# Seven products in place of eight in the second feed-forward layer's up projection

## The reference

```python
def _moe2_ref(x, w_in, w_out, g_ln):       # x: 3072 x 512, w_in: 512 x 1024, w_out: 1024 x 512
    h = x @ w_in
    h_max = np.max(h, axis=-1, keepdims=True)
    e = np.exp(h - h_max)
    sm = e / (np.sum(e, axis=-1, keepdims=True) + 1e-09)
    solu = h * sm
    mu = np.mean(solu, axis=-1, keepdims=True)
    var = np.mean((solu - mu) ** 2, axis=-1, keepdims=True)
    ln = (solu - mu) / np.sqrt(var + 1e-06) * g_ln
    return (ln @ w_out).astype(np.float32)

def reference(...):
    attn_out = _attn_ref(...)               # q, k, v: 4 x 8 x 768 x 64
    x = ...                                 # tokens by features: 3072 x 512
    x = _moe_ref(x=x, ...)                  # gate and value: 512 x 1536 each, out: 1536 x 512
    return _moe2_ref(x=x, ...)
```

## Time and profile before

| | us |
|---|---|
| median of three runs | 971.77 |
| the profiled execution's own time | 974.78 |
| its span, first to last instruction | 972.9 |
| PE busy in the span | 941.5 (97%) |
| DVE busy | 643.6 (66%) |
| ACT busy | 521.7 (54%) |
| POOL busy | 136.1 (14%) |
| stage C, from 697 to the end | 276 |

### The profile page before, as it was taken

One profiled execution on the slowest core, in us unless ns is written; L12 is line 12 of the kernel. 1 busy time (PEld: TensorE's weight loads), 2 busy tenths in 40 slices (PEclk: granted clock), 3 DMA queues, 4 the chain that ended last, 5 costly groups with the idle time before them and its releaser, 6 DMA issues.

```text
span 972.9 us, 14652 instructions
## 1 busy us (share of the span) xinstructions
PE 941.5 (97%) x5334; PEld 832.9 (86%) x5334; DVE 643.6 (66%) x1065; ACT 521.7 (54%) x911; POOL 136.1 (14%) x170
## 2 busy tenths in 40 slices
PE   7979999999999999999999999999999999999996
PEld 4666787787799999999999999999988888888875
DVE  3767885786778755454568877777475775666641
ACT  3554654555555533342546554555477876666632
POOL 4313401101115330000044001010100000000000
PEclk9989999999999999999999999999999999999999
DMA  9746635626153413131374617250520154351533
GB/s 264 215 155 201 183 153 174 184 115 182 55 210 120 157 71 130 49 115 66 111 247 143 229 52 248 87 191 17 170 75 32 27 137 96 88 141 34 112 86 84
DMA packets 103847, 126.61 MB, mean 130 GB/s; under 512 B 8160, under 2 KB 84320, under 8 KB 103776
## 3 DMA queue, kind: packets, MB, share of 16 engines
q1 hardware_dynamic: 98320, 109.28, 36.6%
q0 software_dynamic: 4736, 15.73, 4.7%
q10 hardware_dynamic: 720, 0.66, 0.3%
HBM read 77.41 MB, written 37.75 MB: 118 GB/s over the span
## 4 chain that ended last, share of the span: by engine, by line
PE 79%; DVE 7%; DMA 4%; issue 3%; ACT 3%; SPq 2%; POOL 2%; DVEq 0%; ACTq 0%; POOLq 0%
PE psum L949 10%; PE psum L952 10%; PE psum L951 10%; PE psum L385 8%; PE psum L386 8%; PE psum L387 8%; PE psum L985 6%; PE psum L987 6%; PE psum L988 6%; PE psum L842 3%; PE psum L876 2%; PE psum L866 2%; PE psum L855 2%; DMA w_raw<-weights 1%; DMA v_buf<-v_rows 1%
## 5 line engine op out<-in xcount | busy, mean ns | idle before, releaser
L949 PE MATMUL psum<-xo_hi,w_hi 128*128 128x384 f32 x560 | 195.1, 348 | 7.8 <-DVE psum L1658 2.6
L951 PE MATMUL psum<-xo_lo,w_hi 128*128 128x384 f32 x560 | 188.3, 336 | 0.0
L952 PE MATMUL psum<-xo_hi,w_lo 128*128 128x384 f32 x560 | 188.1, 336 | 0.0
L949 PEld LDWEIGHTS psum<-xo_hi,w_hi 128*128 128x128 f32 x560 | 105.8, 189 | 13.9 <-DVE xo_lo L1644 4.1
L951 PEld LDWEIGHTS psum<-xo_lo,w_hi 128*128 128x128 f32 x560 | 105.9, 189 | 0.8 <-issue 0.3
L952 PEld LDWEIGHTS psum<-xo_hi,w_lo 128*128 128x128 f32 x560 | 105.8, 189 | 0.0
L1163 ACT ACTIVATE xo_hi<-b 128x768 fp32r<-128x768 f32 x84 | 70.6, 846 | 63.2 <-PE psum L988 49.5
L1538 DVE TENSOR_TENSOR xo_lo<-b,xo_hi 128x768 fp32r<-128x768 f32 x84 | 81.2, 969 | 34.5 <-ACT xo_hi L1163 34.3
L385 PE MATMUL psum<-w_out_hi,ln_t_hi 128*128 128x512 f32 x192 | 75.1, 391 | 2.1 <-DVE ln_t_lo L1775 2.1
L1658 DVE TENSOR_TENSOR psum<-psum,p_buf 128x384 f32<-128x384 f32 x48 | 27.1, 564 | 75.0 <-PE psum L952 75.0
L385 PE MATMUL psum<-w_in_hi,x_hi 128*128 128x512 f32 x192 | 75.3, 392 | 0.4 <-ACT h_buf L1284 0.4
(11 more groups left out here) (142 smaller groups left out, 2025.2 us busy)
## 6 DMA issues: line engine op xcount, KB each, us to landing
act_dram<-act_buf SPq DMA_DIRECT2D x48, 384.0 KB, 2.4
b<-act_dram SPq DMA_DIRECT2D x48, 384.0 KB, 4.9
ln_t<-z SPq DMA_DIRECT2D x80, 128.0 KB, 3.1
kq_buf<-k_t SPq DMA_DIRECT2D x32, 192.0 KB, 2.7
kq_buf<-q_t SPq DMA_DIRECT2D x64, 96.0 KB, 3.0
q_dec<-q_t SPq DMA_DIRECT2D x32, 192.0 KB, 2.5
w_raw<-weights POOLq DMA_DIRECT2D x12, 512.0 KB, 4.4
x_dram<-x_tile SPq DMA_DIRECT2D x4, 1536.0 KB, 6.0
```

What stands on the lines that cost most here:

```text
L949: pe.matmul(dst, hi[:, cols], xo_hi[:, i, kc, :], start=i in (P1, P7) and kc == 0, stop=False, skip_group_check=True)
L951: pe.matmul(dst, hi[:, cols], xo_lo[:, i, kc, :], start=False, stop=False, skip_group_check=True)
L952: mm = pe.matmul(dst, lo[:, cols], xo_hi[:, i, kc, :], start=False, stop=kc == HK - 1, skip_group_check=True)
```

## The change

The last seven pairs of blocks (k = 0 to 6, the first is blocks (2,2) and (2,3)) get their up projection by seven products of half size: tokens in two halves (the two blocks), features in two halves, columns in two halves of 512. A product is 2 slices x 3 = 6 matmuls of 512 columns, a pair 42 in place of 48. For it:

- POOL makes four sums of input blocks for each pair (`make_s`, four operations of 128x256, each waiting for the one before), and once, during the gated layer's second round of down products, four sums of weight blocks in eight pieces of 128x512, each stored to DRAM (`sum_t`); the pieces are loaded again by POOL's queue in stage C (`load_t`), two stages of 128x512, and split by ACT and DVE into four weight operands (`t_high`, `t_low`): pieces 0 to 3 in tile 0, pieces 4 to 7 inside the first pair.
- The split of a pair's inputs covers 1792 columns in place of 1024, in three parts (512, 256, 1024).
- PE takes the order P1, P7, P6, P2, P5, then the down projection of one block, then P3, P4, then the down projection of the next. ACT copies P1 from one PSUM bank to another between P1 and P6 (`copy_xy`), and P7 to SBUF (`copy_p7`); DVE adds for P5 and P4 (`add_u3`) and makes one quarter of the result (`add_c22`); ACT copies the other three (`copy_up`).
- Both blocks of a pair are then taken on together: two maxima, two exponents, two normalizations and transposes in a row. One turn buffer `z` holds a tile in place of two.

The core of the diff:

```diff
+        UP_ORDER = (P1, P7, P6, P2, P5, P3, P4)
+        T_PIECES = [(p, a) for p in (P7, P6, P5, P4) for a in range(HK)]
...
+            def up_product(k, i):
+                if i in (P1, P2):
+                    pe.wait_ge(s_lo_ready, 3 * k + 1)
+                else:
+                    pe.wait_ge(s_lo_ready, 3 * k + 3)
+                if k == 0 and i in (P4, P5, P6, P7):
+                    pe.wait_ge(t_lo_ready, T_PIECES.index((i, HK - 1)) + 1)
...
+                elif i in (P6, P2):
+                    pe.wait_ge(up_xy_copied, k + 1)
+                elif i in (P5, P4):
+                    pe.wait_ge(up_u3_ready, k + 1)
+                else:
+                    pe.wait_ge(up_c22_ready, k + 1)
...
                 for j in range(BLOCKS):
-                    if run_up_of(t, j):
-                        both_up(*run_up_of(t, j))
+                    if pair_up(t, j) is not None:
+                        for i in UP_ORDER[0:5] if j % 2 == 0 else UP_ORDER[5:7]:
+                            up_product(pair_up(t, j), i)
                     both_down2(t, j)
...
+            def load_t(i):                       # POOL
+                if i > 1:
+                    pool.wait_ge(t_lo_ready, i - 1)
+                pool.dma_start(t_stage(i)[:], t_store(i)).then_inc(t_loaded[i % 2], DMA)
...
+                    if j % 2 == 0:               # ACT, tiles 1 to 4
+                        if j > 0:
+                            scale_out(t, j - 1)
+                        elif t > 1:
+                            scale_out(t - 1, 3)
+                        ln_high(t, j, 0)
+                        copy_xy(k)
+                        ln_high(t, j, 1)
+                        if k == 0:
+                            for i in (4, 5):
+                                t_high(i)
+                        copy_p7(k)
+                        if k == 0:
+                            for i in (6, 7):
+                                t_high(i)
+                        square_solu(*last_of(k))
+                        deviation_of_pair(last_of(k)[0], last_of(k)[1] // 2)
+                        copy_up(k, P2, UX, 0, 0, up_c11_copied)
+                        if k + 1 < PAIRS:
+                            s_high(k + 1, 0)
+                        continue
                     both_high(t, j)
+                    scale_out(t, j - 1)
+                    copy_up(k, P3, UY, 0, 1, up_c12_copied)
+                    copy_up(k, P4, UV, 1, 0, up_c21_copied)
+                    exponent(*a)
+                    if k + 1 < PAIRS:
+                        s_high(k + 1, 1)
+                        s_high(k + 1, 2)
+                    else:
+                        both_high(*next_block(t, j))
+                    exponent(*b)
+                    square_solu(*a)
...
                     both_low(t, j)
+                    if j % 2 == 0:               # DVE, tiles 1 to 4
+                        if k == 0:
+                            for i in (4, 5):
+                                t_low(i)
+                        add_u3(k)
+                        invert_pair(last_of(k)[0], last_of(k)[1] // 2)
+                        add_c22(k)
+                        turn_up(last_of(k)[0], last_of(k)[1] - 1)
+                        turn_up(*last_of(k))
+                        if k == 0:
+                            for i in (6, 7):
+                                t_low(i)
+                        if k + 1 < PAIRS:
+                            s_low(k + 1, 0)
+                        continue
```

More of the change, by code:

```diff
@@ L227, in retention_moe_kernel @@
             squares = sb(c, "squares", [P, F2])
-            x2_hi0 = sb(c, "x2_hi0", [P, KC, 2 * P], F32R)
+            with ExitStack() as pair:
+                x2_hi0 = sb(pair, "x2_hi0", [P, KC, 2 * P], F32R)
+            up_p7 = sb(c, "up_p7", [P, BANK])
+            sb(c, "gap5", [P, 2 * KC * P - BANK])
             h_buf = sb(c, "h_buf", [P, 2, F2])
@@ L336, in retention_moe_kernel @@
         ln_t_moved = [sem(f"ln_t_moved{i}") for i in range(PARTS)]
+        t_summed = sem("t_summed")
+        t_stored = sem("t_stored")
+        b22_loaded = sem("b22_loaded")
+        t_loaded = [sem(f"t_loaded{i}") for i in range(2)]
+        t_hi_ready = sem("t_hi_ready")
+        t_lo_ready = sem("t_lo_ready")
+        s_made = sem("s_made")
+        s_hi_ready = sem("s_hi_ready")
+        s_lo_ready = sem("s_lo_ready")
+        up_product_done = sem("up_product_done")
+        up_xy_copied = sem("up_xy_copied")
+        up_p7_copied = sem("up_p7_copied")
+        up_u3_ready = sem("up_u3_ready")
+        up_c22_ready = sem("up_c22_ready")
+        up_c11_copied = sem("up_c11_copied")
+        up_c12_copied = sem("up_c12_copied")
+        up_c21_copied = sem("up_c21_copied")
         std_ready = sem("std_ready")
@@ L1019, in up @@
                 mm.then_inc(h_done, 1)
+            def up_product(k, i):
[5 more added lines that the diff above has]
+                    pe.wait_ge(t_lo_ready, T_PIECES.index((i, HK - 1)) + 1)
+                if i == P1:
+                    at_least(pe, up_c11_copied, k)
+                elif i == P7:
+                    at_least(pe, up_c21_copied, k)
+                elif i in (P6, P2):
+                    pe.wait_ge(up_xy_copied, k + 1)
+                elif i in (P5, P4):
+                    pe.wait_ge(up_u3_ready, k + 1)
+                else:
+                    pe.wait_ge(up_c22_ready, k + 1)
+                dst = psum[:, {P1: UX, P2: UX, P7: UV, P4: UV}.get(i, UY), :]
+                for a in range(HK):
+                    x_hi, x_lo = s_hi[:, S_OF[i] * HK + a, :], s_lo[:, S_OF[i] * HK + a, :]
+                    m_hi, m_lo = up_weight(i, a)
+                    pe.matmul(dst, x_hi, m_hi, start=i in (P1, P7) and a == 0, stop=False, skip_group_check=True)
+                    pe.matmul(dst, x_hi, m_lo, start=False, stop=False, skip_group_check=True)
+                    mm = pe.matmul(dst, x_lo, m_hi, start=False, stop=a == HK - 1, skip_group_check=True)
+                mm.then_inc(up_product_done, 1)
             def turn(t, j):
@@ L1314, in square_solu @@
                 act.wait_ge(mean_ready, n + 1)
+                act.wait_ge(squares_summed, {4: 2, 5: 3, 6: 3, 7: 3}.get(n, 4))
                 at_least(act, d_squared, n - BLOCKS)
                 at_least(act, pair_std_ready, 2 * (t - 2) + j // 2 + 1)
-                act.activation(d_squares[:], solu[:, j % 2, :], ACT.Square, bias=mean[:, one],
+                act.activation(squares[:], solu[:, j % 2, :], ACT.Square, bias=mean[:, one],
                                accum_out=squares_sum[:, one]).then_inc(d_squared, 1)
@@ L1423, in stage_c @@
                     copy_h(2, 0, 0)
-                    x2_high(2, 1)
+                    for part in range(3):
+                        s_high(0, part)
                     copy_h(2, 0, 1)
@@ L1864, in stage_c @@
                     take_up(1, 3)
-                    x2_low(2, 1)
+                    for part in range(3):
+                        s_low(0, part)
                     row_max(2, 0)
```

248 lines of the change are left out of this document (203 added, 45 removed).

## The result

With the change the kernel takes 981.46 us, the median of four runs (979.80, 980.24, 982.68, 982.79), against 972.14 for the kernel before in the same comparison: a ratio of 1.0091, with a 95% interval of 1.0067 to 1.0114. It moved by 9.3 us where I had forecast 4.3; the sign was right, and 981.46 lies above the upper end of my range, 980.8.

The account below looks back on a forecast made before the run. PE was taken to bound stage C, though waits set the end. Saved matmuls -9.5, steady pairs +2.5, first pair +8.2, tail +3.1 gave +4.3 us: 971.77 to 976.1 us, range 972.8 to 980.8.

Parts of the forecast that it names:

- The gain: Stage C on PE: seven pairs lose 6 matmuls each, 42 x 0.227 = 9.5 us saved if no new wait appears.
- the 9 that I named as a sign: Profile after the change: PE busy time lower by some 9 us, while stage C is longer by 4.
- The steady pairs: Six steps between pairs: P6 waits for ACT's copy of P1, 0.42 us a pair with restart, 2.5 us in all.
- P6, P5 and P4 of the first pair: PE waits in the first pair for ACT's copy, DVE's sum and the last weight piece: late by 2.4, 1.1 and 3.9 us.
- P3: First pair: P3's sum waits behind ACT's root, which stands behind pieces 6 and 7; late by 0.9 us.
- my own upper bound: First pair's net cost at most 11 us, if turned-block DMAs slow loads by 2 us and POOL's sums slow DVE.
- a cover for POOL's sums: POOL's eight weight sums are hidden in the second round of down products; uncovered they would cost some 6 us.
- The tail: After the last up projection: the chain to the last transpose grows from 9.6 to 12.65 us, all 3.1 counting.
- The turn buffer: One turn buffer in place of two costs nothing: next tile's first transpose comes with 5 us spare.
- That the waits add: First pair: its four waits follow each other on PE and sum to 8.3 us, 8.7 with restarts, net 8.2.
- POOL's sums and DVE: Rival: they collide in every pair, delaying the split P7 waits for, 4.2 us, 980.3; 0.24 together with the slow moves.
- the moves behind a store: Rival: turned-tile moves right behind a store are slow, up to 1 us a tile, 979; 0.24 together with the collision.

Follow-up runs that it names:

- best_2: Changed kernel with early piece loads, first-pair reordering, later squares, last pair's seven products ahead of tile 4's first down projection, POOL's loads behind the input load: 965.39 us.
- squares_late: Changed kernel, with ACT taking the squares of a pair's first block in the next pair, behind the copy of P1: 980.41 us, ratio 1.0088.
- x_late: Changed kernel, with the second pair's 512 KB input load held back until ACT has split all weight pieces: 979.71 us, one run.
- act_order: Changed kernel, with ACT splitting weight pieces 6 and 7 of the first pair after its squares, root and copy of P2: 976.94 us, ratio 1.006.
- early_loads: Changed kernel, with the eight weight pieces loaded as soon as their place is free, splits staying where they were: 975.76 us, ratio 1.0041.
- loads_after_x: Changed kernel, with POOL issuing the weight-piece loads only once the input load that stage C begins with has landed: 980.32 us, ratio 1.0085.
- c22_first: Changed kernel, with DVE making the sum that P3 waits for ahead of the pair's reciprocal: 983.44 us, ratio 1.0115.
- dve_order: Changed kernel, with DVE making the low halves of pieces 6 and 7 ahead of the first pair's normalizations and transposes: 981.2 us, ratio 1.0093.

## Why the prediction was right, and wrong

**The gain.** 42 x 0.227 = 9.5 us. Right: PE's matmuls fell by 42, and best_2, with most of the waits gone, keeps 6.0 of it. PE's busy time fell by 4.9 only and not by the 9 that I named as a sign, since a row in front of a wait counts its full 0.39 us and a row at half clock 0.63.

**The steady pairs**, 2.5 forecast. P6 waits 0.21 to 0.25 in each of six steps (0.31 forecast), with 0.08 of restart each: 1.9 in all. Right in place and cause (squares_late). The other 0.8 of the 2.7 is small restarts elsewhere and one down projection, so that the total came so near is in part luck. In this trace too a table load of 1.28 us is followed by the next instruction 0.02 later (792.41 to 793.71), as in before's. The Trainium skill gives 2.66 us for a switch (ScalarE: Activation LUTs, "What ACT_TABLE_LOAD costs"); by an estimate from it, 1.38 more in each of six steps would have been 8 us, which are not there.

**P6, P5 and P4 of the first pair**, 2.4, 1.1 and 3.9 forecast, 2.33, 1.07 and 3.65 measured. Right.

**P3**, 0.9 forecast, 3.98 measured. This is the step that failed: "takes 0.6 to issue the first and 3.7 from issue to landing: about 789.8 for the second". All of pair 0 came 2.7 us sooner in the profiled execution than in my reckoning, so on its clock I had said 787.1; ACT takes it at 790.63, 3.5 later: 7.0 us from issue to landing, not 3.7. There was a slip of addition too. The terms behind the landing (0.5, 1.19, 1.30, 0.3, 0.2, 0.7) make 4.2, so 794.0 and not the 794.6 that I wrote, and P3 late by 0.3 and not 0.9, the sum +3.7 and not +4.3; the trace has 4.3 from the split to P3. The slip hid 0.6 of the error. The order of instructions was right, and the price of a load was taken from a median over the whole kernel, instead of from the traffic of that stretch: 512 KB from SP and, as far as x_late shows, the moves of a turned tile. act_order and early_loads show that this landing is what P3 waited for. The case stood in my own upper bound ("if DMAs of the turned block slow the loads by 2 us"), where it should have been the value.

**The half clock**, not forecast: five matmuls behind P4's wait at a distance of 0.43, and the restart itself, 1.4 us. The profile of before shows none in stage C, having no wait over 1.3 there; but waits of 3.6 to 4 us had no precedent in its rows, and I priced them at a restart of 0.11.

**The start of the stage**, forecast at nothing, +0.95: pieces 0 and 1 are issued 1.2 us behind an input load for which ACT, and then PE, waits. I named a cover for POOL's sums and none for its loads. loads_after_x takes it away.

**The tail**, 3.1 forecast. The chain from the last up matmul to the last transpose is longer by 3.2, as summed. But PE's end moved by 2.0, not 3.1. From the last up matmul to the start of (5,0)'s down projection it is 17.5 us before and 20.7 after, so up to there the chain counts whole. Then the kernel before waited once more, 1.23 us, for the moves of (5,1); after, PE waits 0.07 there. "All of it counts" left that second wait out.

**The turn buffer**, forecast at nothing, with "5 us spare". That cover isn't there. In the changed kernel DVE waits three times for the moves ahead of a transpose, 3.5 us in all (before, never), and in one pair the wait, followed by a split that falls on POOL's sums, reaches PE:

```profile
881.34 1.25 DVE L2014 STREAM_TRANSPOSE z<-solu 128x1024 f32<-128x1024 f32 x1 [1.71 <-DMA ln_t<-z]
...
885.17 2.36 DVE L2019 TENSOR_TENSOR ln_t_lo<-ln_t,ln_t_hi 128x512 fp32r<-128x512 f32 x2
```

The down projection at 886.45 is 0.4 late with its restart. The split takes 2.36 us in place of 1.28. In the first pair the late pieces hide the wait for the buffer (the transpose starts at 795.54 without one); in act_order, where they don't, it is 2.52 us on DVE, ahead of P4's 2.77 on PE.

**That the waits add.** They do in the sum, and all but P3's were nearly of the right size for that. But c22_first and dve_order show that they are not independent: take one away, and the next takes its time.

With P3 at 4.0 in place of 0.9 (+3.1), the half clock (+1.4), the stage's start (+0.9) and the tail (-1.1) my sum of 4.3 is 8.6, against 8.8 measured in stage C. Of the rivals, none came true: POOL's sums and DVE cost P7 no more than 0.1 a pair and P6 nothing in later pairs, and the moves behind a store are not where the tail is longer (7.6 us from the last transpose to (5,0)'s down projection before, 7.7 after). The two that I put beyond the forecast ended at 979 and 980.3, for other reasons than those that reached 981.5.

## What to carry to other kernels

Before a load is priced at its median, list what every queue issues in the microseconds around it, because a load that lands in 3.1 us alone took 5.4 and 6.5 in company here, and ask which instruction stands first behind it on an in-order engine: here one split of a weight piece held the root of another block, and that held all of DVE. When several waits of one step share a releaser, reordering the engine behind it only moves the wait (dve_order, c22_first); what pays is to have the data there sooner (early_loads), or to take other work ahead of the instruction that waits for it (act_order). A buffer that a change takes away needs its own line in the account: it can be free only as long as something else is later. A change that saves work on the bounding engine should be judged together with its first and its last iteration: six steady pairs cost under 3 us, the first alone over 12.

## What the runs showed of the hardware

**TensorE's clock after waits.** The granted clock in after's trace, in three stretches: P3's matmuls, P4's wait, and P4's first matmuls:

```profile
794.80:796.20 1.40, 1.27 (x6) 1.05 (x6) 1.36 (x2) 1.40 (x4) 1.30 (x1) 0.98 0.00 0
796.20:800.00 3.80, 0.59 (x2) 0.00 (x0) 3.77 (x6) 0.93 (x2) 0.00 (x0) 0.50 0.14 20
800.00:802.50 2.50, 2.46 (x6) 2.01 (x7) 2.50 (x4) 0.00 (x0) 0.00 (x0) 0.50 0.19 75
```

0.50 is the lower level, 1.2 GHz in place of 2.4. It is granted already from the start of P4's wait on; ahead of that stand P3's wait of 3.98 us and 1.2 us of matmuls at the full clock. So the clock fell behind P3's wait, and more than half of the slow stretch passed in P4's. Over the stage C of thirteen traces, PE waited 26 times for 1.2 to 1.95 us, and the granted clock fell in or behind none of these. Of 27 waits of 1.98 us or more, the clock fell inside 6 and within 1.4 us behind 8; five more came while it was low already, and 8 passed without a fall. Each matmul at the lower level costs 0.2 us more. Two traces with nearly the same wait before P6 (2.33 in the changed kernel, 2.31 in dve_order) differ in it, and what decides stays open.

**A load's landing.** A load of 256 KB from POOL lands after 3.7 us as a median in the kernel before, and a piece after 3.1 in the changed kernel with little beside it. Where the moves ran with it, it was taken 5.1 to 5.9 us after its issue (piece 5 in eight traces, and x_late's two), and 5.6 to 7.9 where an input load of 512 KB came as well (pieces 6 and 7 in seven traces), in the changed kernel in a window with the DMA engines full and 257 GB/s. The moves are slowed in turn: the last of the sixteen was waited for until 791.6 in act_order, 6.8 us after its issue.

**DVE beside POOL.** In early_loads the subtraction of pieces 6 and 7 falls on POOL's sums for the next pair, which run from 792.99 to 797.36; in the changed kernel it stands clear of them and takes 1.25 us:

```profile
793.81 1.26 POOL L971 TENSOR_TENSOR s_raw<-s_raw,x_raw 128x256 f32<-128x256 f32 x1
...
793.82 1.80 DVE L2041 TENSOR_TENSOR w_in_lo<-t_stage,w_in_hi 128x512 fp32r<-128x512 f32 x2
```

Both are longer: 1.80 for 1.25 us on DVE, 1.26 for 0.72 on POOL. The Trainium skill (SBUF — State Buffer, "Who interferes with whom") says that the two exclude each other; the rows agree. It was a rival's mechanism, and it is real, but not where the rival had it: in the steady pairs of the changed kernel it reached PE once, at 886, with 0.4 us and behind a wait for the turn buffer.
